# A fused attention and MoE kernel: strided blocks of tokens equal modulo 8, late scales for the first outputs, and part of a weight split moved to GpSimd

## The chip, the core and the metric

The kernel runs on one core of a Trainium2 chip. The metric is the device time of one launch in microseconds, the median of several executions. TensorE does the matmuls, VectorE, ScalarE and GpSimd the elementwise work, SyncE only issues DMAs. The profiler takes one execution; its span is the time from the first to the last instruction.

## The reference, cut

```python
# q, k, v: (4, 8, 576, 64) f32.  Heads 0-3 local, heads 4-7 strided
rel = pos[:, None] - pos[None, :]
mask_local = (rel >= 0) & (rel < 32)
mask_strided = (rel >= 0) & (pos[None, :] % 32 == pos[:, None] % 32)
scores = np.where(masks, scale * q @ k.T, -1e9)
attn = softmax(scores) @ v                       # -> x: (2304, 512)
h = x @ w_in                                     # w_in (512, 2048)
x2 = (h * sigmoid(1.702 * h)) @ w_out            # w_out (2048, 512)
# then a gate with 8 experts: for each token the two best of noisy logits,
out[token] += weight * (relu(x2 @ w1[e]) @ w2[e])
```

## The kernel before, in words

There are three stages: attention (to about 190 us), the first MLP (stage b, to about 575 us) and the experts. The change is in attention and in what is prepared beside it.

Attention works on 16 pairs of heads, `i = 4 b + hp` (batch b, pair hp). Pairs hp 0 and 1 are local, 2 and 3 strided. For a local pair `geometry` gives 6 blocks of 96 queries by 128 keys; for a strided pair 8 blocks of 72 by 72, since a strided head sees only tokens with the same remainder modulo 32. A block holds four neighbouring remainders (18 tokens each), and `mask_s` leaves out the other remainders. `load_v` therefore brings a strided pair's V in 8 DMAs of 36 KB, of 256-byte pieces.

`stage_a` of every engine does one pair after another, with the loads, scores and softmax of later pairs between. On TensorE (line 1606) pair i is: transposes of P for head 0 (`transpose_p`, 1527), transposes of q and k of pair i+2 (`transpose_qk`, 1487), P times V (`p_times_v`, 1546), transposes of P for head 1, scores of pair i+2 head 0 (`scores`, 1498), P times V, scores head 1. Before each P times V four matmuls on constant data (`busy`, 1540, 224 columns, into an unused part of PSUM) fill time. "Pair i starts" below means its first transposes of P (L1536). TensorE's queue is in order.

On VectorE (1098) pair i is: `sums` of pair i+1, `max_and_sub` of pair i+2 head 0 (L998, L1004), `out_lo` of pair i (L1021), `max_and_sub` head 1, then `weights(i)`. ScalarE (772) evacuates transposes (L725 for q and k, L732 for P), does the exponentials (L738) and `out_hi` (L747). GpSimd (570) multiplies P by the reciprocal sums (`norm`, L565). SyncE (418) loads q, k and V of pair i+2 once the scores of pair i are done.

The output x and the weights w_in and w_out are held as two f16 parts, high and low, scaled by a power of two that comes from the largest magnitude. So a maximum must be taken first: `v_max` over all of V, loaded flat (two DMAs of 2.3 MB, lines 406 and 409) into room of the weights; `weights_max` over quarters of w_in and w_out. The maximum of each partition is spread over all partitions by one matmul on TensorE (L1508, in `scores`, the argument `spread`), which waits for the counter `raw_max`; VectorE reads the result in `max_and_sub` (L1000) and makes the scale (`power_of_two`, 978). The four quarters of w_in are looked at in pairs 1 to 4, those of w_out in pairs 9 to 12; the spread is in pairs 5 and 13. Eighths are then split in pairs 6 to 9 (w_in) and 14 to 17 (w_out): `weights_hi` on ScalarE (L769), `weights_lo` on VectorE (L1060), two a pair. At the end of attention `mlp_ahead` starts the first MLP quarters.

```python
MAX_IN, SPLIT_IN, MAX_OUT, SPLIT_OUT = 1, 6, 9, 14
ALL_OF = {0: V_ALL, 1: WG_ALL, MAX_IN + QUARTERS: WI_ALL, MAX_OUT + QUARTERS: WO_ALL}
```

Of the kernel before, what the change touches and what calls it, by code (L numbers as in the profile page):

```python
# [24 lines left out]
P = 128  # L25
# [3 lines left out]
PAIRS = HEADS // 2  # L29
# [6 lines left out]
SRES = 4  # L36
# [32 lines left out]
MAX_IN, SPLIT_IN, MAX_OUT, SPLIT_OUT = 1, 6, 9, 14  # L69
assert (MAX_IN + QUARTERS) % 4 == 1 and (MAX_OUT + QUARTERS) % 4 == 1  # L70
# [6 lines left out]
def program(nc, q, k, v, w_in, w_out, w_gate, w_noise, noise, w1, w2, out):  # L77
    ctx = ExitStack()
    with ctx:
# [188 lines left out]
        def w2_of(par, part, f):  # L268
# [24 lines left out]
            "consts_pool busy_set qk_in0 qk_in1 v_in0 v_in1 v_in2 v_in3 v_flat_in0 v_flat_in1 w_in_in w_out_in "  # L293
            "small_in t_done t_evac s_done mx_done sub_done exp_done sum_done rr_done norm_done pv_done "
            "x1_hi x1_lo raw_max scaled step split_hi split_lo "
# [18 lines left out]

        def is_local(hp):
            return hp < PAIRS // 2

        V_DMAS = [5, 5, 2 * SRES, 2 * SRES]
# [18 lines left out]
        def out_views(b, hp, part):  # L337

            tok = slice(b * SEQ, (b + 1) * SEQ) if isinstance(b, int) else bass.ds(b * SEQ, SEQ)
            dst = x1[:, part, hp, tok]  # L340
            if is_local(hp):
                return [(ps_o[:, :, 0:SEQ // 2], dst.rearrange("p (a x) -> p a x", a=2))]
            dst = dst.rearrange("p (j a x) -> p a j x", j=SLEN, a=2)
            src = ps_o[:, :, 0:SEQ // 2].rearrange("p a (j x) -> p a j x", j=SLEN)
            return [(src[:, a], dst[:, a]) for a in range(2)]

        def load_v(eng, b, hp):
# [41 lines left out]
        def _(sp):  # L389
# [12 lines left out]

            load_qk(0, 0)
            load_qk(0, 1)

            sp.dma_start(w_in_s[:].rearrange("p a c f -> p (a c f)").bitcast(F32)[:, 0:HEADS * SEQ],
                         v[0:2].rearrange("b h (x s) d -> (b h x) (s d)", x=P // (2 * HEADS))
                         ).then_inc(S["v_flat_in0"], 16)
            sp.dma_start(w_out_s[:].rearrange("p a c f -> p (a c f)").bitcast(F32)[:, 0:HEADS * SEQ],
                         v[2:4].rearrange("b h (x s) d -> (b h x) (s d)", x=P // (2 * HEADS))  # L410
                         ).then_inc(S["v_flat_in1"], 16)
            load_v(sp, 0, 0)
            load_v(sp, 0, 1)
# [4 lines left out]
            for i in range(NPAIR - 2):  # L418

                sp.wait_ge(S["s_done"], i * 2 + 2)  # L420
# [102 lines left out]
        def _(pool):  # L523
# [46 lines left out]
            for i in range(NPAIR - 1):  # L570
                for h2 in range(2):
                    norm((i + 1) // PAIRS, (i + 1) % PAIRS, h2)
# [1303 lines left out]
```

## Time and profile before

| | us |
|---|---|
| median of 3 runs | 1030.38 (1029.64 to 1032.16) |
| the profiled execution, time | 1028.2 |
| the profiled execution, span | 1026.4 |
| TensorE busy | 978.1 (95%) |
| VectorE busy | 594.5 (58%) |
| ScalarE busy | 307.6 (30%) |
| GpSimd busy | 219.8 (21%) |

Busy shares are means over stages with different limits. In a timeline row the first number is the start from the span's begin, the second the length; an "x12" merges 12 instructions; the bracket tells how long the engine was idle before and what ended that. In a row of windows the granted clock of TensorE is a share of 2.4 GHz: 1.00 is that level and 0.50 is 1.2 GHz.

### The profile page before, as it was taken

Reading aid. Unit: us, or ns where it says so; the run is one execution under the profiler, and the core shown is the slowest. Engines: PE = TensorE matmul, PEld = TensorE weight load, DVE = VectorE, ACT = ScalarE, POOL = GpSimd, SP = SyncE. Lnnn points to the kernel's source line nnn. Section 1 sums busy time; section 2 is a strip of 40 time slices with the busy share of each in tenths; the row PEclk is TensorE's granted clock in tenths of the full one; section 3 lists DMA queues with packets and bytes.
Section 4 is the critical chain, followed back from the end, with each engine's and each line's share of the span. In section 5 each row is a group of like instructions: output and inputs, shape, how many; then the busy total and the mean of one; then the engine's idle time right before and its main releaser. Section 6 shows DMA issues by size and latency. Waiting matters only on the chain.

```text
span 1026.4 us, 22946 instructions
## 1 busy us (share of the span) xinstructions
PE 978.1 (95%) x9218; PEld 706.8 (69%) x9219; DVE 594.5 (58%) x1033; ACT 307.6 (30%) x427; POOL 219.8 (21%) x274
## 2 busy tenths in 40 slices
PE   7899999999999999999999899989999999999992
PEld 4677777867677576775765767756777767677771
DVE  6588998668777786787887744232232323233231
ACT  2355745523243233332531321111111111111110
POOL 4222323000000000010025124233323333333331
PEclk8699999999999999999999999999999999999997
DMA  9774582097756667567647635848474747475330
GB/s 267 177 187 92 129 196 55 6 393 237 249 204 205 247 214 258 181 205 268 219 149 238 218 78 151 263 114 213 131 210 121 221 120 214 133 209 142 89 82 23
DMA packets 170240, 182.43 MB, mean 178 GB/s; under 512 B 133495, under 2 KB 133495, under 8 KB 167360
## 3 DMA queue, kind: packets, MB, share of 16 engines
q1 hardware_dynamic: 112832, 142.47, 44.6%
q0 software_dynamic: 9600, 27.69, 8.9%
q10 hardware_dynamic: 47744, 11.35, 6.3%
q8 instruction: 48, 0.79, 0.3%
q14 instruction: 16, 0.13, 0.0%
HBM read 116.41 MB, written 53.55 MB: 166 GB/s over the span
## 4 chain that ended last, share of the span: by engine, by line
PE 86%; DVE 4%; DMA 2%; SPq 2%; ACT 2%; issue 1%; POOLq 0%; DVEq 0%; ACTq 0%
PE bank L1760 20%; PE bank L1769 20%; PE bank L1661 18%; PE bank L1586 17%; PE bank L1524 4%; PE bank L1562 3%; PE bank L1494 2%; PE bank L1536 1%; PE bank L1543 1%; PE bank L1513 1%; DMA arena<-out,arena 1%; DMA arena<-in_moe_w 1%; DVE sc L976 1%; SPq L399 1%; ACT arena L725 1%
## 5 line engine op out<-in xcount | busy, mean ns | idle before, releaser
L1586 PE MATMUL bank<-x,w_in_s 128*128 128x256 f16 (+1 forms) x1728 | 194.1, 273 | 2.6 <-DVE x L1021 1.5
L1661 PE MATMUL bank<-w_out_s,arena 128*128 128x512 f16 x864 | 190.2, 379 | 0.0
L1586 PEld LDWEIGHTS bank<-x,w_in_s 128*128 128x128 f16 x1728 | 167.9, 98 | 25.9 <-DVE x L1021 1.8
L1661 PEld LDWEIGHTS bank<-w_out_s,arena 128*128 128x128 f16 x864 | 83.6, 98 | 96.6
L1429 DVE TENSOR_TENSOR arena<-arena 128x512 f32<-128x512 f32 x37 | 25.6, 692 | 161.7 <-ACT arena L899 117.6
L1760 PEld LDWEIGHTS bank<-arena,w_out_s 128*128 128x128 f16 x2016 | 114.5, 98 | 5.9 <-issue 0.8
L1760 PE MATMUL bank<-arena,w_out_s 128*128 128x128 f16 x2016 | 117.0, 219 | 0.6 <-issue 0.6
L1760 PEld LDWEIGHTS bank<-arena,w_in_s 128*128 128x128 f16 x1920 | 109.3, 98 | 5.4 <-issue 0.7
L1760 PE MATMUL bank<-arena,w_in_s 128*128 128x128 f16 x1920 | 111.7, 219 | 0.5 <-issue 0.5
L1769 PE MATMUL bank<-w_out_s,arena 128*128 128x512 f16 x480 | 108.7, 383 | 3.3 <-DVE arena L1424 3.3
L1769 PE MATMUL bank<-w_in_s,arena 128*128 128x512 f16 x480 | 108.6, 383 | 2.3 <-DVE arena L1424 2.3
L1422 DVE CAST arena<-arena 128x512 f16<-128x512 f32 x82 | 35.5, 433 | 124.0 <-ACT arena L894 113.2
L976 DVE TENSOR_REDUCE sc<-arena 128x1 f32<-128x512 f32 (+2 forms) x42 | 100.4, 2404 | 7.6 <-DMA arena<-in_moe_w 4.0
L894 ACT ACTIVATE arena<-bank 128x512 f32<-128x512 f32 x82 | 48.9, 597 | 167.4 <-PE bank L1760 152.3
L1158 DVE SCALAR_TENSOR_TENSOR arena<-arena,sc 128x4096 f16<-128x4096 f32 x16 | 71.7, 4483 | 34.7 <-ACT arena L803 34.7
L1769 PEld LDWEIGHTS bank<-w_out_s,arena 128*128 128x128 f16 x480 | 46.5, 99 | 56.7 <-issue 5.9
L1769 PEld LDWEIGHTS bank<-w_in_s,arena 128*128 128x128 f16 x480 | 46.5, 99 | 55.8 <-issue 2.8
L899 ACT ACTIVATE arena<-bank,arena 128x512 f32<-128x512 f32 x40 | 27.5, 687 | 185.9 <-PE bank L1769 182.7
L803 ACT ACTIVATE arena<-arena,sc 128x4096 f16<-128x4096 f32 x16 | 59.3, 3709 | 61.9 <-DVE sc L985 61.9
L632 POOL DMA_INDIRECT arena<-out,arena x37 | 44.2, 1196 | 130.7 <-DMA out<-arena 116.6
L565 POOL TENSOR_TENSOR arena<-arena 96x768 f32<-96x768 f32 (+1 forms) x32 | 44.2, 1397 | 124.8 <-DVE arena L1015 124.7
L637 POOL DMA_INDIRECT out<-arena x40 | 41.4, 1034 | 104.5 <-DVE arena L1429 98.4
(196 smaller groups left out, 992.8 us busy)
## 6 DMA issues: line engine op xcount, KB each, us to landing
arena<-in_moe_w SPq DMA_DIRECT2D x16, 2048.0 KB, 11.5
split_weights<-arena SPq DMA_DIRECT2D x16, 2048.0 KB, 7.4
w_in_s<-split_weights SPq DMA_DIRECT2D x32, 512.0 KB
w_out_s<-split_weights SPq DMA_DIRECT2D x32, 512.0 KB
arena<-in_q SPq DMA_DIRECT2D x32, 144.0 KB, 3.6
arena<-in_k SPq DMA_DIRECT2D x32, 144.0 KB, 3.7
out<-zeros SPq DMA_DIRECT2D x1, 4608.0 KB, 25.1
x_rows<-arena SPq DMA_DIRECT2D x18, 256.0 KB, 3.3
```

The lines of the kernel that those rows point to most:

```text
L565: pool.tensor_tensor(pr, pr, rr[hp % 2][0:nq, h2, 0:nb].unsqueeze(2).to_broadcast([nq, nb, nk]), ALU.mult).then_inc(S["norm_done"], 1)
L632: pool.indirect_dma_start(out=prior[b4 % 2], out_offset=None, in_=out, in_offset=bass.IndirectOffsetOnAxis(ap=cur[b4], axis=0), bounds_che ...
L637: pool.indirect_dma_start(out=out, out_offset=bass.IndirectOffsetOnAxis(ap=cur[b4], axis=0), in_=ysb[b4 % 2], in_offset=None, bounds_check ...
L803: nc.scalar.activation(halves[:, 0], raw[m], ACT.Copy, scale=col(S_U + m)).then_inc(S["unit_hi"], 1)
L894: nc.scalar.activation(hf[half], ps_dh[half], ACT.Relu, scale=DOWN).then_inc(S["relu_done"], 1)
L976: return nc.vector.tensor_reduce(dst, src, AX.X, ALU.max, apply_absolute_value=True)
L1158: nc.vector.scalar_tensor_tensor(halves[:, 1], raw[m], col(S_U + m), halves[:, 0], ALU.mult, ALU.subtract).then_inc(S["unit_lo"], 1)
L1524: last = mm(dst, ql, kr, start=False, stop=True, skip_group_check=True)
L1586: last = mm(dst, w_in_s[:, w_part, c, f * P:(f + 1) * P], x1[:, x_part, c, tok], start=(c == 0 and w_part + x_part == 0), stop=(c == DC - ...
L1661: last = mm(ps_x[j], g[par][:, g_part, f, j * P:(j + 1) * P], w_out_s[:, w_part, f], start=(n == 0), stop=(n == 3 * FC - 1))
L1760: last = mm(ps_dh[half][:, n * P:(n + 1) * P], w1_of(w_par, w_part, c, f), xt[par][:, x_part * DC + c], start=(c == 0 and w_part + x_part ...
L1769: last = mm(ps_y[par], h[par][:, h_part, f * P:(f + 1) * P], w2_of(w_par, w_part, f), start=(n == 0), stop=(n == 3 * EFC - 1))
```

## The change

**Blocks.** A strided block now holds the 72 tokens with the same remainder modulo 8, which contain four remainders modulo 32. Token 8p + n is row p of block n. V of a strided pair comes in one DMA (2 KB pieces), and q, k and the output are permuted by other strides in the evacuations.

**Order of the loads.** V's flat loads come in four parts, with pairs 0 to 3; q and k of pair i+2 are loaded as soon as the transposes that used their tile are done; V of pairs 0 and 1 is issued by ScalarE.

**Late scales.** Pairs 0 to 3 copy their output as f32 into room of x that is used later (`held_out`); pairs 4 to 7 make its high and low part beside their own. V's maximum is needed only by pair 4.

**Maxima and splits.** V's maximum is taken in pairs 0 to 2, the first three quarters of w_in in pairs 3 to 5, of w_out in pairs 10 to 12; the last quarter in pairs 6 and 13, ahead of `max_and_sub`. w_in is split in pairs 7 to 10, and GpSimd makes every second low part (two instructions: it multiplies the raw values, then subtracts the high part).

**Fillers.** TensorE gets fillers of 512 columns between its first pieces of work, loses the four ahead of head 0's P times V, and gets one of 256 columns ahead of each of the four groups of q and k transposes. These go to the scores' PSUM, so a wait for VectorE's subtraction of the next pair comes first.

```diff
@@ SyncE
             load_qk(0, 0)
             load_qk(0, 1)
...
-            load_v(sp, 0, 0)
-            load_v(sp, 0, 1)
+            sp.wait_ge(S["t_done"], 4)
+            load_qk(0, 2)
+            load_v_flat(0)
+            sp.wait_ge(S["t_done"], 8)
+            load_qk(0, 3)
+            load_v_flat(1)
...
-            for i in range(NPAIR - 2):
-
-                sp.wait_ge(S["s_done"], i * 2 + 2)
+            for i in range(2, NPAIR - 2):
+
+                sp.wait_ge(S["t_done"], 8 * i - 2)
                 load_qk((i + 2) // PAIRS, (i + 2) % PAIRS)
+                if i == 2:
+                    load_v(sp, 0, 2)
+                    load_v(sp, 0, 3)
+                if i <= 3:
+                    load_v_flat(i)
+                sp.wait_ge(S["pv_done"], 2 * i - 2)
                 load_v(sp, (i + 2) // PAIRS, (i + 2) % PAIRS)
@@ load_v, strided
-                s = s.rearrange("h (j g r) d -> h r j g d", j=SLEN, g=SB)
-                for h2 in range(2):
-                    for r in range(SRES):
-                        eng.dma_start(vn[hp][r:SQ:SRES, :, h2], s[h2, r]).then_inc(v_in[hp], 16)
-
+                eng.dma_start(v_tile(hp)[0:SQ].rearrange("p h n d -> p h (n d)"),
+                              s.rearrange("h (p n) d -> p h (n d)", n=SB)).then_inc(v_in[hp], 16)
@@ GpSimd
+            def w_in_lo(n):
+                e = 2 * n
+                pool.wait_ge(S["split_hi"], e + 1)
+                pool.tensor_scalar(eighth_raw(e), eighth_raw(e), col(S_WI), None, ALU.mult
+                                   ).then_inc(S["scaled_pool"], 1)
+                pool.wait_ge(S["scaled_pool"], n + 1)
+                pool.tensor_tensor(eighth(w_in_s, 1, e), eighth_raw(e), eighth(w_in_s, 0, e), ALU.subtract
+                                   ).then_inc(S["split_lo_pool"], 1)
+
@@ ScalarE, evacuation of q and k, strided
-                    dst = dst.rearrange("c (g a j r) -> c a j g r", g=SB, a=2, j=SLEN // 2)
-                    src = src.rearrange("c a (j g r) -> c a j g r", g=SB, r=SRES)
+                    dst = dst.rearrange("c (n a p) -> c a p n", n=SB, a=2)
+                    src = src.rearrange("c a (p n) -> c a p n", n=SB)
@@ ScalarE, out_hi
-                if i == 0:
+                if b == 0:
+                    for src, dst in out_views(b, hp, None):
+                        last_op = nc.scalar.activation(dst, src, ACT.Copy)
+                    last_op.then_inc(S["x1_lo"], 1)
+                    return
...
+                if b == 1:
+                    act.wait_ge(S["x1_lo"], 2 + hp)
+                    nc.scalar.activation(x1[:, 0, hp, 0:SEQ], held_out[hp], ACT.Copy, scale=col(S_V)
+                                         ).then_inc(S["late_hi"], 1)
@@ ScalarE, start
             evac_qk(0, 0, 0)
             evac_qk(1, 0, 1)
+            load_v(act, 0, 0)
             evac_qk(2, 1, 0)
             evac_qk(3, 1, 1)
             exps(0, 0, 0)
             exps(0, 0, 1)
+            load_v(act, 0, 1)
@@ VectorE, out_lo
+                if b == 1:
+                    dve.wait_ge(S["late_hi"], hp + 1)
+                    nc.vector.scalar_tensor_tensor(x1[:, 1, hp, 0:SEQ], held_out[hp], col(S_V), x1[:, 0, hp, 0:SEQ],
+                                                   ALU.mult, ALU.subtract).then_inc(S["late_lo"], 1)
@@ VectorE, stage_a
                     if i == 0:
-                        v_max(3)
-                        dve.wait_ge(S["step"], steps[0])
-                        absmax(col(V_MAX), col(PART_MAX, 4)).then_inc(S["raw_max"], 1)
+                        v_max(0)
+                    if i == SPLIT_IN - 1:
+                        weights_max(S["w_in_in"], QUARTERS - 1)
+                    if i == SPLIT_OUT - 1:
+                        weights_max(S["w_out_in"], QUARTERS - 1)
                     weights_lo(i, 0)
                     if more2:
                         max_and_sub(b2, hp2, 0, ALL_OF.get(i))
@@ TensorE
+            def transpose_qk(n, hp, which, loads, idle=0):
...
                 for a in range(2):
+                    busy(idle, slice(0, 2 * P), ps_s[0][:, 0])
...
-                busy(4, slice(SEQ // 2, 4 * P))
+                if h2 == 1:
+                    busy(4, slice(SEQ // 2, 4 * P))
...
             transpose_qk(1, 0, 1, 16 * QK_DMAS)
+            busy(2)
...
             scores(0, 0, 0, 2)
+            busy(2)
             scores(0, 0, 1, 2)
+            busy(2)
...
+            busy(2)
             scores(0, 1, 0, 4)
+            busy(2)
             scores(0, 1, 1, 4)
+            busy(4)
...
+                    spread = (V_MAX, b + 2) if hp == 0 and not last else (B_MAX, 2 * b + 2) if hp == 2 else None
+                    if hp == 1 and last:
+                        spread = (B_MAX, 7)
...
                     if more:
-                        transpose_qk(k[1], hp2, 0, loads)
+                        pe.wait_ge(S["sub_done"], i * 2 + 3)
+                        transpose_qk(k[1], hp2, 0, loads, 1)
+                        transpose_qk(k[2], hp2, 1, loads, 1)
...
-                        scores(b2, hp2, 0, k[2] + 1,
-                               (V_MAX, 1) if hp == 0 else (B_MAX, b + 2) if hp == 1 else None)
+                        scores(b2, hp2, 0, k[2] + 1, spread)
```

## Rows read from the trace of the kernel before

**Rows 1.** The page's part 2: granted TensorE clock in 40 equal slices, in tenths.

```profile
PEclk8699999999999999999999999999999999999997
```

**Rows 2.** Windows: stretch, length, busy us (instructions) by engine, clock, DMA.

```profile
13.00:15.00 2.00, 1.13 (x8) 0.70 (x8) 1.61 (x3) 1.68 (x5) 0.00 (x0) 1.00 1.01 433
15.00:17.30 2.30, 2.30 (x13) 2.03 (x12) 2.30 (x2) 0.96 (x2) 0.00 (x0) 0.62 0.97 417
28.70:35.20 6.50, 6.45 (x34) 5.18 (x34) 3.84 (x5) 3.28 (x7) 2.81 (x2) 0.50 0.37 71
42.50:44.00 1.50, 1.50 (x18) 1.13 (x16) 0.82 (x1) 0.52 (x1) 0.00 (x0) 0.88 0.20 44
92.67:102.80 10.13, 9.68 (x98) 7.90 (x97) 9.17 (x17) 6.70 (x14) 2.29 (x2) 1.00 0.44 97
```

**Rows 3.** Timeline of the start: start us, us, engine, line, operation [idle before].

```profile
11.47 5.91 SPq L351 DMA_DIRECT2D arena<-in_v  x1
...
20.93 1.22 PE L1536 MATMUL bank<-ident,arena 96*128 96x96 f32 x6
...
28.71 2.46 PE L1494 MATMUL bank<-ident,arena 96*128 96x96 f32 x12 [6.56 <-DMA arena<-in_k]
...
44.01 0.71 PE L1536 MATMUL bank<-ident,arena 96*128 96x96 f32 x6
```

**Rows 4.** Who TensorE waited for, 0 to 190 us: total, times, longest.

```profile
PE bank L1494 <- DMA arena<-in_k: 6.6, 1, 6.6
PE bank L1494 <- ACT arena L725: 3.6, 15, 0.3
```

**Rows 5.** Timeline of pairs 5 and 6, from the last quarter of w_in on.

```profile
83.21 0.71 PE L1536 MATMUL bank<-ident,arena 96*128 96x96 f32 x6
...
84.78 2.27 DVE L976 TENSOR_REDUCE sc<-arena 128x1 f32<-128x2048 f32 x1
...
87.91 0.22 PE L1508 MATMUL bank<-identb,sc 128*128 128x128 bf16 x1
...
92.00 0.82 DVE L1021 SCALAR_TENSOR_TENSOR x<-bank,sc,x 128x576 f16<-128x576 f32 x1 [0.78 <-ACT x L747]
...
92.67 0.69 PE L1536 MATMUL bank<-ident,arena 72*72 72x72 f32 x8
...
95.18 0.55 PE L1543 MATMUL bank<-busy_in 128*128 128x224 bf16 x4
...
95.66 1.22 PE L1562 MATMUL bank<-arena 72*64 72x72 f32 x16
...
96.49 2.31 POOL L565 TENSOR_TENSOR arena<-arena 72x576 f32<-72x576 f32 x2 [6.03 <-DVE arena L1015]
...
97.33 0.49 PE L1513 MATMUL bank<-arena,identb 96*96 96x384 bf16 x2
...
97.63 2.25 DVE L1060 SCALAR_TENSOR_TENSOR w_in_s<-arena,sc,w_in_s 128x1024 f16<-128x1024 f32 x1
...
100.78 0.95 DVE L1004 TENSOR_TENSOR arena<-bank,arena 96x768 f32<-96x768 f32 x1
...
104.77 1.27 DVE L1060 SCALAR_TENSOR_TENSOR w_in_s<-arena,sc,w_in_s 128x1024 f16<-128x1024 f32 x1
```

**Rows 6.** Timeline of TensorE near 670 us, at a later hole.

```profile
670.49 7.03 PE L1769 MATMUL bank<-w_out_s,arena 128*128 128x512 f16 x24 [3.28 <-DVE arena L1424]
```

**Rows 7.** The chain that ended last: 24 such matmuls, undisturbed.

```profile
682.89 5.18 PE bank L1769 x24
```

**Rows 8.** Timeline of pair 13, around the spread of w_out's maximum.

```profile
165.62 0.74 DVE L1013 TENSOR_REDUCE arena<-arena 72x8 f32<-72x576 f32 x1
...
166.44 0.22 PE L1508 MATMUL bank<-identb,sc 128*128 128x128 bf16 x1
...
167.24 0.20 DVE L1015 RECIPROCAL arena<-arena 72x8 f32<-72x8 f32 x1
```

**Rows 9.** Groups of instructions by shape, 0 to 190 us.

```profile
L725 ACT ACTIVATE arena<-bank 128x288 f32<-128x288 f32 x64 | 22.6, 404 | 20.0 <-PE bank L1494 19.9
```

More of the change, by code:

```diff
@@ L68 @@
 BUSY = 12
-MAX_IN, SPLIT_IN, MAX_OUT, SPLIT_OUT = 1, 6, 9, 14
-assert (MAX_IN + QUARTERS) % 4 == 1 and (MAX_OUT + QUARTERS) % 4 == 1
+SPLIT_IN, SPLIT_OUT = 7, 14
 CONSTS = 6 + 4 + SLEN + 1
@@ L312, in program, with v_tile @@
         w_ready = [S["w_even"], S["w_odd"]]
+        v_flat = [t[:].rearrange("p a c f -> p (a c f)").bitcast(F32)[:, 0:HEADS * SEQ] for t in (w_in_s, w_out_s)]
+        held_out = [x1[:, 0, hp, 2 * SEQ:4 * SEQ].bitcast(F32) for hp in range(PAIRS)]
         def is_local(hp):
             return hp < PAIRS // 2
-        V_DMAS = [5, 5, 2 * SRES, 2 * SRES]
+        V_DMAS = [5, 5, 1, 1]
+        def v_tile(hp):
+            return vn[hp].rearrange("p n h d -> p (n h d)").rearrange("p (h n d) -> p h n d", h=2, n=SB)
         def geometry(hp):
@@ L401, in load_qk, with load_v_flat @@
                                      ).then_inc(qk_in[par], 16)
+            def load_v_flat(n):
+                half = HEADS * SEQ // 2
+                at = slice(n % 2 * half, (n % 2 + 1) * half)
+                rows = v[n // 2 * 2:n // 2 * 2 + 2].rearrange("b h (x s) d -> (b h x) (s d)", x=P // (2 * HEADS))
+                sp.dma_start(v_flat[n // 2][:, at], rows[:, at]).then_inc(S[f"v_flat_in{n}"], 16)
             load_qk(0, 0)
             load_qk(0, 1)
[L406 to L411, printed above, removed]
-            load_v(sp, 0, 0)
-            load_v(sp, 0, 1)
+            sp.wait_ge(S["t_done"], 4)
[4 more added lines that the diff above has]
+            load_v_flat(1)
             sp.dma_start(wg[:, :, 0:E], w_gate.rearrange("(c p) e -> p c e", p=P)).then_inc(S["small_in"], 16)
@@ L989, in _ @@
             nc.vector.memset(zeros[:], 0.0).then_inc(S["zero_done"], 1)
[L990 to L991 removed]
+            for c in (V_MAX, B_MAX):
+                nc.vector.memset(col(c), 0.0).then_inc(S["raw_max"], 1)
             def max_and_sub(b, hp, h2, all_of=None):
@@ L1057, in weights_lo @@
                     n = (i - first) * 2 + half
-                    if 0 <= n < 2 * QUARTERS:
+                    if 0 <= n < 2 * QUARTERS and not (before == 0 and half == 0):
                         dve.wait_ge(S["split_hi"], before + n + 1)
@@ L1485, in _, with busy @@
             mm = nc.tensor.matmul
-            def transpose_qk(n, hp, which, loads):
+            def busy(n, columns=slice(0, 4 * P), ps=ps_busy):
+                for _ in range(n):
+                    mm(ps[:, columns], busy_in[:, 0:P], busy_in[:, P:P + columns.stop - columns.start],
+                       start=True, stop=True, skip_group_check=True)
+            def transpose_qk(n, hp, which, loads, idle=0):
                 pe.wait_ge(qk_in[hp % 2], loads)
@@ L1538, in transpose_p @@
                     last.then_inc(S["t_done"], 1)
-            def busy(n, columns=slice(0, 4 * P)):
-                for _ in range(n):
-                    mm(ps_busy[:, columns], busy_in[:, 0:P], busy_in[:, P:P + columns.stop - columns.start],
-                       start=True, stop=True, skip_group_check=True)
             def p_times_v(n, b, hp, h2, v_use):
@@ L1560, in p_times_v @@
                     else:
-                        o = o.rearrange("p (j n r) -> p n j r", j=SLEN, n=half)[:, m % half]
-                    last = mm(o, vn[hp][0:nk, m, h2], pt[0:nk, m * nq:(m + 1) * nq], start=True, stop=True)
+                        o = o.rearrange("p (k n) -> p n k", n=half)[:, m % half]
+                    values = vn[hp][0:nk, m, h2] if is_local(hp) else v_tile(hp)[0:nk, h2, m]
+                    last = mm(o, values, pt[0:nk, m * nq:(m + 1) * nq], start=True, stop=True)
                 last.then_inc(S["pv_done"], 1)
```

91 lines of the change are left out of this document (48 added, 43 removed).

## The prediction

> **What bounds the kernel now.** I read the page first: TensorE's clock is granted in full in nearly all of 40 slices, not in the first two [rows 1]. The windows of the start show where [rows 2]: full up to 15.0, 0.62 on the mean to 17.3 (so it falls near 15.5), at the lower level of 1.2 GHz (0.50) from 28.7 to 35.2, and back only inside 42.5 to 44.0. The waits of TensorE over the attention stage name one hole, 6.6 us until keys arrive; the others are holes of 0.2 to 0.3 us before the transposes of q and k, 3.6 us in 15 pieces [rows 4]. The timeline of the start shows the cause [rows 3]: SyncE sits 5.91 us in one issue of V, behind the two flat loads of V (2.3 MB each), before it comes to the q and k that TensorE needs at 22.15 and gets at 28.71. From the second pair on (44.01 [rows 3]) the work is even: a pair takes 9.46 us (83.21 to 92.67 [rows 5]) or 10.13 us, 9.68 of them busy on TensorE [rows 2]. There TensorE is the bound, and VectorE, 9.17 of 10.13, is close behind it.
>
> **Part 1, the start.** V's flat loads are cut in four and spread over four pairs, q and k of pair 2 are issued as soon as the first transposes free their tile (near 8 us), and the V blocks of pairs 0 and 1 go out from ScalarE. The 6.6 us hole goes. Next, the clock. Before, it fell behind the stretch from 13 to 15 us, in which TensorE was busy 1.13 of 2.0 us [rows 2]. The 14 new fillers of 512 columns stand in just those gaps, so I take it that the clock holds. One costs 0.22 us: four of 224 columns take 0.48 with their start [rows 5], some 0.1 each, and 512 columns are 2.3 times as many. VectorE no longer takes a V maximum ahead of the first sums, so the first transposes of P wait for TensorE's own queue alone. That queue works from 15.5 to 20.93 at half clock now; at full clock the 5.4 us are 2.7, and the 12 fillers that fall behind the first scores put 2.6 back: 20.8 against 20.93 [rows 3]. Nothing is gained to that point; but pair 0 then takes 9.46 us instead of 23.1, so pair 1 starts at 30.3 instead of 44.01: 13.7 us. ScalarE now issues ten DMAs, five behind its first evacuations and five just ahead of pair 0's. An issue can hold its engine for 5.91 us when the queues are full [rows 3], but with V's flat loads cut up they are fuller later, not here. The first five lie under scores, the second five have some 4 us until the next evacuation is due. I charge 0.2 us, range 0 to 4. **Start: -13.5, range -14 to -8**; the small end is that the clock falls as now: from 28.71 to 44.01 TensorE spent 15.3 us, less 1.2 of waiting, on what takes 9.46 - 0.95 = 8.5 in pair 5 (0.71 of transposes and a hole come before it [rows 4, 5]), so the low spell cost 5.6.
>
> **Part 2, the even stretch.** Each pair loses one block of four fillers (95.18 to the next work at 95.66: 0.48 us [rows 5]) and gets four single ones of 256 columns, 0.11 us each, ahead of the four groups of q and k transposes. Two fall into the holes of 0.2 to 0.3 us that are there [rows 4]; two delay work that had no hole, 0.2 us with issue. Net -0.3 us a pair, between 0 and -0.48. It counts in 12 pairs; in the two with a stall (part 3) it is eaten, in the last two nothing is put back, so they give -0.48 each. **-3.6 and -1.0.** The fillers lie in the scores' PSUM, so the first waits for VectorE's subtraction of the next pair: that ends at 101.73, and the transposes come 0.95 us into the pair that starts at 102.80, 2 us later [rows 2, 5]; what is queued behind it (both q/k transposes, P times V) waits only if VectorE lags by more.
>
> The strided blocks (equal modulo 8 instead of four neighbours of a period of 32) change strides only. The mask is the same pattern. V comes in one DMA instead of eight, SyncE's issue shortens, but no wait of TensorE after 28.7 us is for a DMA [rows 4]: 0. The evacuation of q and k now writes elements 288 bytes apart instead of runs of four. The row that holds both of its present layouts, contiguous and in runs of four, has one mean, 404 ns for 288 columns, over 64 of both kinds [rows 9]: nothing in it hangs on the stride. I take 0; were it twice as long, TensorE would wait 0.35 us more in some links of half the pairs, +6.
>
> **Part 3, the maxima of the weights.** This is what costs. Now VectorE takes a quarter's maximum (2.27 us for 128x2048) at the end of a pair, and the matmul that spreads the result finds it ready: the last quarter runs from 84.78 to 87.05, and TensorE passes at 87.91 without waiting [rows 5]. In the changed code the last quarter stands behind the sums and in front of the maximum and subtraction, in pairs 6 and 13, and TensorE's scores of the same pair wait for it. Queued behind that wait: two scores, both P times V, all of the next pair. The third quarter moves to the end of the pair before, so VectorE is also late when it starts.
> Pair 6, on the old clock: pair 5's low part ends at 92.82, + the new late low part, 0.79 (1024 columns took 1.27 at 104.77, less 0.15 of start, times 576/1024, plus the start) = 93.6; + maximum and subtraction, 2 x 0.75 (0.95 for 768 columns at 100.78) = 95.1; + third quarter 2.27 = 97.4; + two sums, 1.8 (in pair 13 from 165.62 to 167.44 [rows 8]) = 99.2; + the last quarter 2.27 and the maximum of four, 0.2 = 101.7. TensorE reaches the scores at 97.33 [rows 5]: 4.4 us idle. VectorE also brings a lag from pair 4, which gets V's scale and a late part too: 2.2 (sums) + 3.1 + 0.9 (scale) + 0.8 + 0.8 + 2.3 = 10.1 us of work in 9.2; up to 0.9 more. I take 4.7, range 3.5 to 5.5. Pair 13: a quarter's maximum stands ahead of the sums already now, as the third will, and they end at 167.44; + 2.5 = 169.9 against 166.44 [rows 8]: 3.5, with a lag out of pair 10 (which has both a w_out quarter and a low eighth) 4.0, range 3 to 5. **+8.7, range +6.5 to +10.5.**
>
> Does the clock fall there? Behind a hole of 3.28 us later in the kernel, 24 matmuls took 7.03 instead of 5.18 us [rows 6, 7]: 1.85 us lost. Both new holes are longer. In the attention stage the clock came back more slowly: 6.45 busy of 6.5 us from 28.7 did not bring it [rows 2], and that spell cost 5.6. So a fall costs 1.85 to 5.6; I take 3.0 at pair 6, 2.5 at pair 13 (dense matmuls follow sooner). **+5.5, range 0 to +11.**
>
> **Part 4, GpSimd makes half of the low eighths.** VectorE loses one instruction of 1.27 to 2.25 us in pairs 7 to 10 [rows 5]; GpSimd gets two of 128x1024. Nearest row: two norms of 72x576 in 2.31 us, so 2.1 each, 4.1 us a pair. GpSimd now works 2.29 of 10.13 us [rows 2], and its norms for the next pair end at 98.8, 4 us before TensorE asks at 102.80 [rows 5]: hidden. If that cover were gone a norm would start up to 1 us late. SyncE waits for both engines before it loads w_out, two pairs ahead of its use: 0. But VectorE's operation with two SBUF inputs took 2.25 us beside a GpSimd norm and 1.27 alone [rows 5]: its end is what it would be had it begun when the norm ended. So GpSimd's 4.1 us can push VectorE's remaining eighth and the strided pair's sums by 1 us; the slack of 2 us takes it: 0, at worst +1 in each of four pairs.
> The Trainium skill, GPSIMD Engine Reference, section 4.1 (Engine selection), speaks against this part: elementwise work belongs on VectorE, GpSimd being about twice as slow with two inputs. The trace agrees in size (1.15 us for 576 columns against VectorE's 0.95 for 768 [rows 5]), and the sum is the same by either, because GpSimd is idle three quarters of a pair. SBUF — State Buffer, section "SBUF: two separate sides", calls the pair of ports an exclusive lock for a whole instruction; the 2.25 us row fits that, and by that rule the at-worst case above is the one to expect for every overlap.
>
> **Part 5, late scales.** Pairs 0 to 3 drop VectorE's low part (0.8) and pairs 4 to 7 get it beside their own, with a 0.7 us copy on ScalarE. ScalarE works 6.70 of 10.13 us [rows 2]: hidden. On VectorE it is the 0.79 already counted in part 3.
>
> **The sum.** -13.5 - 3.6 - 1.0 + 8.7 + 5.5 = -3.9 us. The profiled execution had a span of 1026.4 and a time of 1028.2 us; the median of three is 1030.38, and I put the difference on the median: 1026.5.
>
> **Rivals.** (A) The clock survives the two holes: for it, the 6.6 us hole came when the clock was already down, so none shows a fall in this stage; against it, the 3.28 us row. Without the 5.5: 1021; with the holes at their lower bounds and the fillers nearly free, 1017. (B) The start is not won whole: fillers or ScalarE's issues fail and the clock falls near 15 us as now; for it, that the clock fell with TensorE still busy more than half of the time. +5.6 and 0.5 for fillers at half clock: 1032.6. (C) Each fall costs 5.6: 1032. (D) Slower: the clock stays down after pair 6. One of two filler blocks is gone and the single ones replace its columns only, while with both blocks the low spell lasted from 15.5 to past 42.5 us. A low spell costs 0.44 us per us (5.6 in 12.6 of work). My sum includes 5.5, some 12 us of low clock in all; slower by over 0.3% needs 28 us of it, and 34 us (three pairs and a second fall) give 9.5 over the sum: 1036. (E) The fillers do not do what they say, no saving in part 2: 1030.
>
> **Chances.** Forecast 0.43 (of it 0.27 below 1027.3), A 0.25, C and E 0.17, B 0.09, D 0.06. A measurement of this kernel tells 0.3%, about 3 us, from no change. Faster by more: 0.27 + 0.25 + 0.02 = 0.54. Within: 0.16 + 0.12 + 0.03 = 0.31. Slower: 0.03 + 0.06 + 0.06 = 0.15. The range goes from A's lower end to just above B: 1017 to 1034; the forecast's own is 1022 to 1031.
>
> **What would show it.** Start: no idle window at 22 us, full clock through 40 us, first transposes of P near 20.8 and of pair 1 near 30.3. Even stretch: pairs of 9.2 and 9.8 us. Stalls: TensorE's spreading matmul waits for VectorE's small maximum twice, 5 and 4 us, with low clock behind each. GpSimd: four pairs with 4 us more and no TensorE wait for a norm. I am wrong if the two waits are absent or under 3 us, if the clock holds behind them, or if pair 1 starts after 34 us.

## The result, and the profile after

| | before | changed |
|---|---|---|
| median | 1030.01 (4 runs, 1024.26 to 1032.16) | 1058.88 (4 runs, 1046.21 to 1069.52) |
| ratio, 95% interval | | 1.018 [1.011, 1.026] |
| the profiled execution, time and span | 1028.2, 1026.4 | 1046.21, 1044.6 |
| granted clock, mean of the span | 0.976 | 0.962 |

The ratio compares only executions within 1.5% of the fastest of their kernel; by the medians the changed kernel is 2.8% slower. Its four times go with its clock: 0.962, 0.960, 0.939 and 0.938. The kernel was forecast at 1026.5; it is slower, and outside the range.

In the trace all of the loss lies in attention. I read the start first, in the timeline of TensorE (columns as in [rows 3]).

```profile
21.13 0.66 PE L1591 MATMUL bank<-ident,arena 96*128 96x96 f32 x6
...
30.65 0.71 PE L1591 MATMUL bank<-ident,arena 96*128 96x96 f32 x6
```

Pair 1 starts at 30.65, where it started at 44.01 [rows 3]: the 13.4 us of the forecast are there. Pair 14 starts at 192.19, where it started at 171.20, and from there to the end the traces take 852.4 us (changed) and 855.2 us (before). So 34.4 us were lost between pair 1 and pair 14. Who TensorE waited for, 0 to 220 us (total, times, longest, as [rows 4]):

```profile
PE bank L1563 <- DVE sc L1011: 7.5, 2, 4.2
PE bank L1538 <- DMA arena<-in_k: 6.9, 3, 4.4
PE bank L1549 <- ACT arena L749: 2.2, 7, 0.3
```

The first row is the wait for the weights' maxima; the second is new and was not forecast: waits for keys, in pairs 5, 9 and 11. Windows over pairs 5 to 13 (each line one pair, from its first transposes to the next pair's; length, busy us by engine, clock, DMA):

```profile
69.43:82.65 13.22, 11.83 (x94) 9.59 (x92) 9.14 (x12) 7.14 (x14) 2.27 (x2) 0.74 0.95 157
82.65:101.62 18.97, 14.56 (x100) 11.44 (x98) 12.15 (x17) 5.46 (x13) 2.25 (x2) 0.65 0.27 64
101.62:112.70 11.08, 11.08 (x97) 9.40 (x96) 7.67 (x16) 7.97 (x15) 5.92 (x4) 0.82 0.00 0
112.70:122.28 9.58, 9.13 (x94) 7.29 (x94) 9.44 (x13) 7.91 (x13) 4.63 (x3) 1.00 0.23 74
122.28:137.89 15.61, 11.26 (x94) 9.24 (x92) 7.11 (x11) 7.66 (x13) 11.33 (x7) 0.78 0.96 209
137.89:147.76 9.87, 9.71 (x99) 7.85 (x97) 7.60 (x13) 6.76 (x14) 6.94 (x5) 1.00 0.66 160
147.76:165.52 17.76, 16.62 (x97) 13.76 (x96) 10.25 (x13) 5.34 (x12) 4.24 (x3) 0.56 0.84 181
165.52:176.40 10.88, 10.88 (x93) 8.94 (x93) 8.45 (x10) 6.04 (x11) 2.93 (x2) 0.77 0.03 8
176.40:192.19 15.79, 12.08 (x96) 9.30 (x94) 10.36 (x14) 5.43 (x11) 2.25 (x2) 0.78 0.00 1
```

Before, each of these took 9.46 to 10.14 us at a clock of 1.00. Only pairs 8 and 10 do so now. The five waits stand in these rows:

```profile
71.54 0.37 PE L1538 MATMUL bank<-busy_in 128*128 128x256 bf16 x1 [1.39 <-DMA arena<-in_k]
...
91.40 0.27 PE L1563 MATMUL bank<-identb,sc 128*128 128x128 bf16 x1 [4.24 <-DVE sc L1011]
...
127.35 0.37 PE L1538 MATMUL bank<-busy_in 128*128 128x256 bf16 x1 [4.35 <-DMA arena<-in_k]
...
149.59 0.27 PE L1538 MATMUL bank<-busy_in 128*128 128x256 bf16 x1 [1.14 <-DMA arena<-in_k]
...
184.65 0.26 PE L1563 MATMUL bank<-identb,sc 128*128 128x128 bf16 x1 [3.25 <-DVE sc L1011]
```

Against the lengths of before, pairs 5, 6, 7, 9, 11, 12 and 13 take 3.8, 8.8, 1.0, 6.1, 7.6, 1.4 and 6.3 us more: 34.9. Of these 7.5 are waits for VectorE and 6.9 waits for keys; the other 20.5 us are the same work at the lower clock: by the rows above the clock is at 0.50 for some 59 us of these pairs, 54 of them outside the holes, so I estimate 0.38 us for each us. After the hole of 1.14 us, for one, pair 11 has next to no idle time and takes 17.76 us at a clock of 0.56. The remaining six pairs together win 0.6 us.

Why the keys are late is in SyncE's queue. Its waits (total, times, longest), and its timeline:

```profile
SPq L443 <- POOL w_in_s L587: 16.2, 1, 16.2
...
SPq L445 <- DVE w_in_s L1104: 9.6, 3, 4.1
...
SPq L438 <- DMA arena<-in_moe_w_in: 7.4, 1, 7.4
```

```profile
55.08 8.59 SPq L438 DMA_DIRECT2D arena<-in_moe_w_in  x2
63.71 0.98 SPq L402 DMA_DIRECT2D arena<-in_q  x2
64.74 1.92 SPq L402 DMA_DIRECT2D arena<-in_k  x2
...
118.46 0.38 SPq L445 DMA_DIRECT2D arena<-in_moe_w_out  x1
118.89 1.05 SPq L402 DMA_DIRECT2D arena<-in_q  x2
119.98 2.88 SPq L402 DMA_DIRECT2D arena<-in_k  x2
```

Two quarters of w_in are issued in one step, and the second waits until the first has landed (7.4 us, L438): q and k of pair 7 stand behind them and go out at 63.71 to 66.66, together with that second megabyte. TensorE asks for them in pair 5, at 70.15, and has them at 71.54. Later SyncE waits for both engines' low eighths, issues 1 MB of w_out, and right behind it, at 118.89 to 122.86, q and k of pair 11; TensorE asks for these in pair 9, at 123.00, and has them at 127.35.

### The profile page after: what moved, and what is told of

The parts are those of the page before. It is cut to its first block, busy times and chain, and to the rows that moved or that the text cites. A ratio compares the mean times of both kernels' runs of the same rounds, so it can differ in the third digit from the quotient of the medians.

```text
span 1044.6 us, 22924 instructions
## 1 busy us (share of the span) xinstructions
PE 995.7 (95%) x9222; PEld 719.1 (69%) x9224; DVE 588.1 (56%) x1029; ACT 317.5 (30%) x431; POOL 238.5 (23%) x282
## 4 chain that ended last, share of the span: by engine, by line
PE 83%; DVE 5%; DMA 4%; SPq 3%; ACT 2%; issue 1%; POOL 1%; ACTq 0%; POOLq 0%
PE bank L1821 20%; PE bank L1830 20%; PE bank L1722 17%; PE bank L1643 16%; PE bank L1579 3%; PE bank L1613 2%; DMA arena<-in_k 2%; DMA arena<-in_moe_w_in 1%; SPq L402 1%; PE bank L1549 1%; PE bank L1538 1%; DVE sc L1011 1%; PE bank L1591 1%; DMA arena<-in_moe_w 1%; PE bank L1568 1%
## 5 line engine op out<-in xcount | busy, mean ns | idle before, releaser
L661 POOL DMA_INDIRECT out<-arena x40 | 41.7, 1042 | 106.3 <-DVE arena L1477 99.6
```

Of the source, the lines that this page charges most:

```text
L661: pool.indirect_dma_start(out=out, out_offset=bass.IndirectOffsetOnAxis(ap=cur[b4], axis=0), in_=ysb[b4 % 2], in_offset=None, bounds_check ...
```

## The experiments

Every kernel below also carries one register operation on TensorE's table read; the last experiment shows what it costs. "Pair 14" is the start of pair 14 in the trace: 171.20 before, 192.19 changed.

**1. Keys ahead of the weights in SyncE's queue.** The weight quarters, each with its waits (`load_weights`), are issued one pair later, behind the next q and k.

```diff
             for i in range(2, NPAIR - 2):
                 sp.wait_ge(S["t_done"], 8 * i - 2)
                 load_qk((i + 2) // PAIRS, (i + 2) % PAIRS)
+                load_weights(i - 1)
...
-                for n in ([0], [1], [2, 3])[i - 2] if i < 5 else []:
```

> The changed kernel (fast runs near 1048 us), with one difference on SyncE: the loads of w_in and w_out quarters are issued one pair later, behind the next q and k (and w_in's last two quarters in two pairs instead of one), so that no q or k stands behind a weight load. Theory A (the queue): the three waits of TensorE for keys, 6.9 us in all, are q and k issued late behind 1 MB loads and behind SyncE's wait for a split; each wait also drops the clock. Expected: those waits gone, the clock full in pairs 5, 9 and 11, about 1031 us (17 less). Rival B (the fillers): the clock falls in this stage because half of the fillers are gone, whatever the holes: only the waits go, about 1041 us, and the low spells stay somewhere else.

1039.80 us (10 runs), ratio 1.008 [1.004, 1.013]; pair 14 at 180.29. No wait for keys is left, pairs 5, 9 and 11 take 9.79, 9.53 and 9.81 us at the full clock, and 11.9 us of the 21 are back, though only 6.9 were waits. Both waits for maxima stay. So theory A holds for what the queue does. Its time does not: 1039.8 is rival B's number, not 1031. In this trace the clock stays low behind pair 6's wait for 33 us instead of 14, which makes pairs 7 and 8 8.0 us longer than in the changed kernel, and the part from pair 14 on takes 860.6 us instead of 852.4, for a reason that is open.

**2. Maxima one pair earlier.** The quarters' maxima go to the ends of pairs 2 to 5 and 9 to 12, none ahead of `max_and_sub`.

```diff
-                if 3 <= i < SPLIT_IN - 1:
-                    weights_max(S["w_in_in"], i - 3)
+                if i == 2:
+                    dve.wait_ge(S["raw_max"], 3)
+                if 2 <= i < SPLIT_IN - 1:
+                    weights_max(S["w_in_in"], i - 2)
...
-                    if i == SPLIT_IN - 1:
-                        weights_max(S["w_in_in"], QUARTERS - 1)
```

> The changed kernel with the maxima of the weights one pair earlier: w_in's four quarters at the ends of pairs 2 to 5, w_out's at the ends of pairs 9 to 12, so that nothing stands between the sums and the scores' spread in pairs 6 and 13. Theory A: the two waits of TensorE for VectorE's small maximum (4.24 and 3.25 us) go, and with them the low clock behind them: pairs 6 and 13 shorten by 8.8 and 6.3, about 1033 us. Rival B: only the waits go, 7.5 us: 1040 us. Rival C: VectorE gets late by the moved maxima and the waits come back before other work: 1045 or more.

1033.56 us (10 runs), ratio 1.003 [1.000, 1.006]; pair 14 at 177.29. TensorE's waits, 0 to 175 us:

```profile
PE bank L1536 <- DMA arena<-in_k: 7.3, 3, 3.3
...
PE bank L1561 <- DVE sc L1011: 0.3, 1, 0.3
```

The 7.5 us of waiting for VectorE are gone and 14.9 us are won; the time is theory A's. Behind the three waits for keys the clock still falls.

**3. Both.**

> Both repairs together: q and k ahead of the weight loads, and the maxima one pair earlier. Theory A (holes drop the clock): with no hole of TensorE left in pairs 0 to 13 the clock stays full, a pair takes 9.5 and 9.8 us throughout, pair 14 starts near 156 us (171.20 before, 192.19 in the changed kernel) and the time is about 1015 us. Rival B (one filler block is too little even without a hole): the clock still falls somewhere in pairs 1 to 13, pair 14 starts after 165 us.

1019.26 us (4 runs), ratio 0.989 [0.983, 0.995]; pair 14 at 160.83. The two repairs win 31.4 us in attention, more than 11.9 + 14.9. This kernel beats the one before. Pair 14 was expected near 156. One spell of low clock is left in this trace, behind two small waits in pair 4, which takes 12.39 us instead of 9.6:

```profile
60.55 0.71 PE L1591 MATMUL bank<-ident,arena 96*128 96x96 f32 x6 [0.48 <-POOL arena L580]
61.88 0.39 PE L1538 MATMUL bank<-busy_in 128*128 128x256 bf16 x1 [0.62 <-DVE arena L1042]
...
65.88:67.88 2.00, 2.00 (x14) 1.78 (x13) 1.93 (x4) 0.75 (x3) 0.96 (x1) 0.50 1.01 343
```

**4. What the low clock alone costs.** Experiment 1 again, with TensorE kept busy on constant data inside its two waits for VectorE; the loop over the batches is written out.

```diff
-            with pe.Fori(0, BATCH - 1) as b:
+            for b in range(BATCH - 1):
                 stage_a(b)
...
                     if more:
+                        busy({SPLIT_IN - 1: 40, SPLIT_OUT - 1: 32}.get(i, 0), slice(SEQ // 2, 4 * P))
                         scores(b2, hp2, 0, k[2] + 1, spread)
```

> Prices the clock alone. Taken from the kernel with q and k ahead of the weights in SyncE's queue (1039.8 us; first pair 14 matmul at 180.29, clock low from 87 to past 116 us and again from 173): TensorE gets 40 fillers of 224 columns ahead of the spreading matmul in pair 6 and 32 in pair 13, some 3.8 and 3.0 us, which lie inside its waits of 4.24 and 3.27 us; its loop over the batches is written out so that only these two places get them. VectorE, and so the end of both waits, stays as it is. If the low clock behind the waits is what costs most (theory 1), the clock holds, the waits themselves remain (TensorE passes near 87.2 again) and pair 14 starts near 168 to 170, the time falls to about 1028. If the loss is the waits and VectorE's lateness alone (rival), pair 14 starts within 2 us of 180 and the time stays near 1040.

1024.05 us (7 runs), ratio 0.994 [0.991, 0.996]; pair 14 at 164.22. The same place in experiment 1, and with the wait filled (TensorE's timeline, then windows from the end of the wait; both kernels):

```profile
87.24 0.27 PE L1565 MATMUL bank<-identb,sc 128*128 128x128 bf16 x1 [4.24 <-DVE sc L1013]
...
97.46 1.17 PE L1593 MATMUL bank<-ident,arena 72*72 72x72 f32 x8
```
```profile
87.24:119.00 31.76, 31.76 (x168) 25.68 (x169) 15.61 (x27) 12.90 (x24) 7.86 (x4) 0.50 0.11 28
...
120.00:122.00 2.00, 2.00 (x20) 1.66 (x19) 1.13 (x2) 2.00 (x5) 1.74 (x2) 0.86 0.94 337
```
```profile
83.17 4.00 PE L1540 MATMUL bank<-busy_in 128*128 128x224 bf16 x40
87.58 0.22 PE L1565 MATMUL bank<-identb,sc 128*128 128x128 bf16 x1 [0.41 <-DVE sc L1013]
...
93.10 0.69 PE L1593 MATMUL bank<-ident,arena 72*72 72x72 f32 x8
```
```profile
87.58:108.00 20.42, 19.81 (x188) 15.77 (x188) 16.00 (x28) 13.64 (x27) 7.90 (x4) 1.00 0.19 45
```

Writing the loop out changes nothing that is seen: pairs 0 to 5 are within 0.02 us of those of experiment 1. In both, TensorE passes 8.75 us after pair 6 began: the wait is the same. Behind it the clock is at 0.50 for 33.3 us in the one (to 120.6, by the mean of 0.86 in the last row) and at 1.00 in the other. From pair 6 to pair 9 they take 47.6 and 33.6 us: the fall cost 13.9, or 0.42 us for each us at 1.2 GHz (the forecast had 0.44). The Trainium skill, TensorE: Matmul & The Clock Gate, section "HAM oscillation — how this bites in real kernels", counts half of the throttled time, 16.7 here; the measured price is somewhat lower. Pair 13 takes 15.5 and 13.0: 2.5. The whole, 16.1 us in the trace and 15.8 by the medians, is clock, more than the 10 to 12 that I expected of it. The waits themselves, 7.5 us, are still in a kernel that is faster than before.

**5. The old strided blocks in the repaired kernel**, and **6. in the changed one.** The layout of four neighbouring remainders and V in eight DMAs are put back, with the matching strides of q, k and the output.

```diff
-                    dst = dst.rearrange("c (n a p) -> c a p n", n=SB, a=2)
-                    src = src.rearrange("c a (p n) -> c a p n", n=SB)
+                    dst = dst.rearrange("c (g a j r) -> c a j g r", g=SB, a=2, j=SLEN // 2)
+                    src = src.rearrange("c a (j g r) -> c a j g r", g=SB, r=SRES)
```

> As the kernel with both repairs, but strided blocks and V's loads of strided pairs as before (eight DMAs of 256-byte pieces; q and k evacuated in runs of four). In the changed kernel an evacuation of a strided pair's q or k takes 0.6 us of ScalarE instead of 0.4, and pairs 0 and 1 of a batch take 9.52 instead of the 9.2 that the fillers alone give. If the stride of the writes is the cause: these pairs shorten by 0.3 us, eight times in all 2.5 us, unless the eight DMAs hold SyncE and make q or k late again (holes, 3 us or more slower).

> The changed kernel with the old blocks alone (runs of four neighbours out of 32 tokens, V in eight loads). In the repaired kernel a strided pair took 9.53 us where the old blocks took 9.08 (first two head pairs; 9.86 against 9.75 in the other two), so the new blocks cost 0.28 us a pair on the mean, 4 us in all. If that holds here (theory 1), pairs at full clock are 9.1 and 9.75 us and both weight waits remain: pair 14 starts near 188 and the time is 3 us less, about 1055. If the eight V loads in SyncE's queue delay q and k further (rival), the waits for keys grow by 3 us each and the time is 1060 to 1070.

In the repaired kernel: 1023.62 us (10 runs), ratio 0.996 [0.994, 0.998]. The evacuation of q and k, 80 to 160 us, with the new blocks and with the old (ns min/median/max):

```profile
L751 ACT ACTIVATE arena<-bank x32: 393/543/764, 84.2 to 154.8; 128x288 f32<-128x288 f32 x32
```
```profile
L753 ACT ACTIVATE arena<-bank x33: 393/410/411, 83.7 to 159.9; 128x288 f32<-128x288 f32 x33
```

So the stride does cost: up to 764 ns where q and k are strided, 0.4 us as before where they are local or in runs of four. TensorE waits for it 2.8 us in 9 pieces instead of 0.7 in 2, and pairs 0 and 1 of a batch, in which strided q and k are transposed, take 9.53 us against 9.08 (149.39 to 158.47). The other pairs take 9.8 to 9.9 us in both. But the old blocks bring another hole. In the kernel of experiment 5 TensorE stands 4.9 us at 54.33 for GpSimd, GpSimd for VectorE, and VectorE for data:

```profile
49.51 2.55 DVE L1015 TENSOR_REDUCE sc<-w_out_s 128x1 f32<-128x2304 f32 x1 [8.40 <-DMA w_out_s<-in_v]
```

That is V's flat part, queued behind 16 small V loads, which hold SyncE for 13.10 us in both kernels (from 30.44 in experiment 5, from 29.19 in experiment 6). Behind that wait the clock is at 0.50 until about 75 us, and pairs 2 and 3 take 14.87 and 17.46 us. In the changed kernel the old blocks cost more: 1067.51 us (4 runs), ratio 1.038 [1.033, 1.043], 8.1 us of waiting for keys instead of 6.9, and a wait of 3.4 us for GpSimd at 53.03. The strided blocks, which look like a matter of strides only, bring V in one load instead of eight, and by these traces that is what lets the new order of the loads work; layout and loads were only ever put back together, so the two are not told apart by a run. Neither expected gain (2.5 and 3 us) came.

**7. Fillers.** Head 0's four fillers put back in the changed kernel, in the repaired one, and taken out of the kernel before:

```diff
-                if h2 == 1:
-                    busy(4, slice(SEQ // 2, 4 * P))
+                busy(4, slice(SEQ // 2, 4 * P))
```

> The changed kernel with the four fillers put back ahead of head 0's P times V (the single ones stay), so that each pair has both blocks as before. Theory A: the clock falls behind holes whatever the fillers: the low spells stay, and 14 blocks of 0.48 us make it slower: 1052 us or the same. Rival B: the missing block is why a hole of 1.1 to 1.4 us drops the clock and why it stays low for 10 to 20 us: the low spells shorten or go, 1030 to 1038 us.

> As the kernel with both repairs, and head 0's four fillers back. Theory A: nothing is left for them to protect in pairs 0 to 13; each costs 0.4 us, 14 times: pair 14 starts 5 to 6 us later, 1020 us; only the short low spell behind the 1.1 us hole of pair 14 can go. Rival B: the clock needs them, and this one is the faster of the two.

> The kernel before, only head 0's four fillers taken out. It has TensorE holes of 1.21 us (at 36 us) and 1.10 us (pair 14, 173 us) and none between. Theory F (the fillers decide whether a 1.1 us hole drops the clock): behind the 1.10 us hole the clock now falls as in the changed kernel (0.58 there, 1.00 before), and 14 blocks of 0.48 us are saved where the clock is full: about 1026 us. Rival: the clock holds behind that hole and the time is 1023 us. If the clock falls in pairs 2 to 13, where there is no hole over 0.3 us, the block is needed for the even stretch itself, and the time is over 1030.

| | median | ratio |
|---|---|---|
| changed, both blocks | 1051.18 (4 runs) | 1.022 [1.015, 1.028] |
| repaired, both blocks | 1020.05 (10) | 0.993 [0.990, 0.996] |
| before, one block | 1027.61 (10) | 0.995 [0.990, 0.999] |

With both blocks the changed kernel's waits for keys in pairs 5 and 11 shrink to 0.72 and 0.76 us, the clock holds behind them, and these pairs take 10.5 and 10.8 us instead of 13.2 and 17.8: low spells go, as rival B said, though here the holes are shorter too. But a wait for keys of 2.95 us appears in pair 12, the clock falls behind each wait of 2.86 to 3.85 us, and after the one of 3.85 us it stays down for 15.6 us, as without (14.2): theory A's time. In the kernel before, a block less makes the pairs 9.08 and 9.75 us long instead of 9.47 and 10.13: 0.39 each. The clock falls for 3.4 us behind the 1.10 us hole of pair 14, as theory F said, and the times scatter more (1015 to 1042). In the repaired kernel both blocks cost nothing that can be measured: each pair is 0.4 us longer, but in its trace the low spell of pair 4 is not there.

**8. GpSimd's part undone**, VectorE making all low eighths again, in the changed and in the repaired kernel:

```diff
-                if SPLIT_IN <= i < SPLIT_IN + QUARTERS:
-                    w_in_lo(i - SPLIT_IN)
...
-                    if 0 <= n < 2 * QUARTERS and not (before == 0 and half == 0):
+                    if 0 <= n < 2 * QUARTERS:
```

> The changed kernel with the low eighths of w_in all on VectorE again; SyncE then waits for VectorE alone. GpSimd needs 5.0 us a pair for its two instructions. Theory A: SyncE's wait ahead of w_out is ended late by either engine, and the order of the queue is the cause: within 4 us of the changed kernel. Rival G: GpSimd's slowness is what makes q and k late in pairs 9 and 11: those two waits (5.5 us) and their low clock go, about 1034 us.

> From the kernel with both repairs (q and k first, maxima one pair early: 1019.26 us): GpSimd's part undone, VectorE makes all low eighths. If GpSimd's part is worth its cover (theory 1: hidden, and VectorE has slack now), nothing measurable: 1018 to 1021. If GpSimd's 5 us a pair hold up VectorE (rival), 1 us in each of four pairs is won: 1015. If VectorE needs the relief, small holes in pairs 7 to 10 with a clock fall: 1024 to 1030.

1050.13 us (4 runs; 1041.14 to 1060.98) in the changed kernel, whose eight times are 1046 to 1070. The wait for keys in pair 9 is 2.58 us instead of 4.35, since SyncE no longer waits for GpSimd; the other four are the same. In the repaired kernel 1021.05 us (6 runs), ratio 0.992 [0.988, 0.996], against 0.989 [0.983, 0.995] with GpSimd's part: no difference. In the changed kernel's trace pair 14 comes 3.0 us earlier without it, of the 21.0 that were lost: GpSimd's share is a small part of the loss, and worth nothing where it does no harm.

**9. The changed kernel again.**

> The changed kernel once more, for a second trace and more times (its four times so far were 1046.21, 1049.41, 1068.36 and 1069.52 us with clocks of 0.962, 0.960, 0.939 and 0.938). Its only edit is one register operation on TensorE's table read, which every experiment here carries. If the clock is what scatters (theory 1), the waits for VectorE and for keys are the same as before within 1 us, every time has its clock (about 1 us more for each 0.001 less), and the median lies between 1046 and 1070. If the waits themselves differ from execution to execution (rival), the sum of the five waits, 14.4 us, is another one by more than 3 us. If the register operation costs anything, pairs 0 to 4 take more than 9.52 and 9.87 us.

1053.22 us (4 runs), ratio 1.023 [1.014, 1.032]. Maxima 7.5 us and keys 7.7 us of waiting, pairs 1 to 3 of 9.52, 9.87 and 9.82 us: the waits repeat within 0.8 us, and the register operation costs nothing that is seen. The times are 1048.80, 1067.04, 1048.15 and 1057.63 at clocks of 0.964, 0.941, 0.963 and 0.950, some 0.8 us for each 0.001. By these clocks, what scatters is how long the clock stays down; no trace of this kernel shows an execution at 0.94, so in which pairs it stays down longer is open. From pair 14 on this trace takes 855.6 us, where the first took 852.4.

## Why the prediction was wrong

By its own steps, in us, for the changed kernel's trace:

| step | forecast | measured |
|---|---|---|
| start | -13.5 | -13.4 |
| even stretch, to pair 14 | -3.6 | -0.6 |
| waits for VectorE's maxima | +8.7 | +7.5 |
| waits for keys | 0 | +6.9 |
| clock | +5.5 | +20.5 |
| from pair 14 on | -1.0 | -2.8 |
| sum, span | -3.9 | +18.2 |

The medians differ by 28.9; the 11 us beyond the trace are in the executions with the lower clock. The -2.8 from pair 14 on is no gain of the change: the second trace of the same kernel has +0.4 there, and five traces whose program is the same in that part (the changed kernel twice, experiments 1 to 3) lie between 852.3 and 860.6 us. Of the 22.1 us between forecast and measured span, 18.9 belong to the first step below, 3.0 to the second and 3.0 to the even stretch; the waits for maxima and the part from pair 14 on give 3.0 back.

**The start** was right, point by point: first transposes of P at 21.13 (20.8), pair 1 at 30.65 (30.3), clock 1.00 until pair 5. Which of its parts kept the clock (fillers, or keys in time) no run tells. The reading of [rows 4] was short: the small holes ahead of the q and k transposes are 7.0 us in 28 pieces, not 3.6 in 15, and two holes of 1.21 and 1.10 us stand beside the one named; no term of the sum changes by it.

**The waits for maxima** were right in place, cause and size: 4.24 and 3.25 us against 4.7 and 4.0. The lag out of earlier pairs that was added did not come.

**The first step that failed** is in part 4: "SyncE waits for both engines before it loads w_out, two pairs ahead of its use: 0." I asked when w_out is needed, and not what stands behind that wait in SyncE's queue. Q and k of the pair after next do, and they are needed within a few us. The same holds for "([0], [1], [2, 3])", two quarters of w_in in one step, the second waiting for the first; I did not price it. Together they are 6.9 us of waiting, and 12.0 us of the clock's 20.5 lie behind them by the windows: 2.4 in pair 5, 1.8 in pair 9, 7.8 in pairs 11 and 12. Experiment 1 gave back 11.9 of these 18.9; the rest is the longer fall behind pair 6 in its trace (8.0).

**The second** is the size of the clock's term, in part 3: 3.0 us at pair 6 and 2.5 at pair 13. Pair 13 was right (2.5, experiment 4). The fall behind pair 6's wait cost, by the windows, 5.5 in the changed kernel, where the clock came back at 105.6, and 13.9 in experiment 1. The two foreseen falls are 8.5 us in the changed kernel's trace, within the range of 0 to 11; it is the upper bound that the experiment refutes, and without the holes for keys the kernel, at 1039.8 us, would still have been outside the forecast. I set the upper bound at 5.6 because the one long low spell that the trace of before had cost that. But that was one spell; its length was not a bound, and nothing in the profile said when it would end. Why the same wait is followed by 14 us of low clock in four traces and by 33 in one stays open. And the 12.0 us behind the holes for keys had no place in the sum, since those holes were taken to be none: 1.14 us of waiting drew 7.8 us behind it.

**The third**, smaller, is in part 2: "nothing in it hangs on the stride". The row had one mean for two layouts, contiguous and runs of four; neither is single elements 288 bytes apart. A mean over layouts that are fast says nothing of one that it doesn't hold. The net saving by the fillers was right (a block is 0.39 a pair, experiment 7; with the single fillers the net is 0.39 and 0.32, 9.08 and 9.81 in experiment 5 against 9.47 and 10.13), and the slower evacuation takes it back in half of the pairs.

**Rivals.** D had the direction (slower, the clock staying down after pair 6, 0.44 us for each us), and experiment 1 shows a spell near its 34 us, 33.3; that the lengths agree is luck. Its condition, that one filler block is gone, is not what the long falls hang on: with both blocks the clock falls as well behind 3.9 us. C had the mechanism with 5.6 a fall, and both lacked the keys. E was partly true, for another reason. GpSimd's instructions took 2.86 and 2.13 us, not twice 2.1, and were hidden from TensorE, but not from SyncE.

## What to carry to other kernels

Before a wait on the queue of an engine that issues DMAs is priced at nothing, list what stands behind it in that queue and when it is needed; the moved load's own due time is the wrong question. In a stretch of small matmuls such as this one a hole can be paid twice, and the second price, the low clock, was up to seven times the first (1.14 us, then 7.8); a trace without such holes gives no upper bound for it. So either remove the hole or fill it with work on constant data, which here turned 1039.8 into 1024.1 us with the wait still in it. When a change is a bundle, its parts are worth what they are together: its layout cost 0.4 us in half of the pairs, yet without the layout and its single load of V the new order of loads was worse.

## What the runs showed of the hardware

The same 1.10 us hole at pair 14 left the clock at 1.00 in the kernel before and in the repaired kernels of experiments 3, 5 and 7, and took it to 0.50 for 3.4 to 6.8 us in the changed kernel, in experiments 1, 2, 4, 6, 8 and 9, and in the kernel before with one filler block. The kernel before, and the same with one filler block:

```profile
172.99 1.47 PE L1586 MATMUL bank<-x,w_in_s 128*128 128x256 f16 x12 [1.10 <-DVE arena L1004]
```
```profile
169.56 2.27 PE L1587 MATMUL bank<-x,w_in_s 128*128 128x256 f16 x12 [1.10 <-DVE arena L1004]
```

So with one filler block a pair the clock fell behind this hole in nine of eleven traces, with both in none of two: the fillers may lower the odds, and they do not decide alone. A later hole of 1.51 us, ahead of 144 matmuls of 256 columns in a row, left the clock at 1.00 in all fourteen traces (here the kernel before with one filler block):

```profile
190.60 15.89 PE L1587 MATMUL bank<-x,w_in_s 128*128 128x256 f16 x144 [1.51 <-DVE x L1021]
```

Holes of 0.48 and 0.62 us, 0.7 us apart, took the clock down in experiment 3 (61.5 to 68.3 us); single ones of 0.60 and 0.63 us, 10 us apart, did not in experiment 8. The length of a hole alone doesn't tell whether the clock falls, nor for how long: holes of 4.24 us, with the same kind of work behind them, were followed by 14 us at 1.2 GHz in four traces (the changed kernel twice, experiments 6 and 8) and by 33.3 us in experiment 1, though TensorE was busy throughout (31.76 of 31.76 us to 119.00).

ScalarE writes 288 f32 elements per partition that lie 288 bytes apart in up to 0.76 us, in runs of four or contiguous in 0.41.

GpSimd's multiplication with one tensor input took longer than its subtraction with two:

```profile
109.57 2.86 POOL L584 TENSOR_SCALAR arena<-arena,sc 128x1024 f32<-128x1024 f32 x1
112.51 2.13 POOL L587 TENSOR_TENSOR w_in_s<-arena,w_in_s 128x1024 f16<-128x1024 f32 x1
```

The Trainium skill, GPSIMD Engine Reference, section 4.1 (Engine selection), calls one-input operations roughly line-rate and those with two inputs some two times slower than VectorE. The trace is near the second (2.13 us, where VectorE's low part of the same size, also with two inputs, took 1.27 [rows 5]); it does not bear out the first in so far as the one-input instruction was the longer of the two. No run has it on VectorE. And beside that second row VectorE's late low part (128x576) took 2.60 us, from 112.66, where it took 0.81 alone; its end, 115.26, is 0.62 us behind GpSimd's (114.64), as if it had begun about then.
